# Values products of attention one half step later, beside the scores of a later unit

## The reference, cut to what matters

```python
# x: attention output, (2304 tokens, 512); batch 4, 8 heads, seq 576, head_dim 64
scores = scale * np.matmul(q, k.transpose(0, 1, 3, 2))
mask_local = (rel >= 0) & (rel < stride)                    # heads 0 to 3, stride 32
mask_strided = (rel >= 0) & (pos[None, :] % stride == pos[:, None] % stride)   # heads 4 to 7
scores = np.where(masks[None, :, :, :], scores, -1000000000.0)
attn = np.exp(scores - np.max(scores, axis=-1, keepdims=True))
attn = attn / (np.sum(attn, axis=-1, keepdims=True) + 1e-09)
x = np.matmul(attn, v)                                      # heads side by side
h = x @ w_in                                                # 512 to 2048
g = np.where(h >= 1, h, np.where(h <= -1, 0.0, (h + 1) ** 2 / 4.0))
y = g @ w_out                                               # 2048 to 512
out = y.copy()                                              # then, where y @ w_skip > 0:
e_idx = np.argmax(y @ w_gate, axis=1)                       # one of 8 experts
out += gate_w * (np.maximum(y @ w1[e_idx], 0.0) @ w2[e_idx])
```

## Time and profile before

| | |
|---|---|
| time, median of 3 runs (lowest to highest) | 545.35 us (545.23 to 545.76) |
| the profiled execution's own time | 546.15 us |
| its span | 541.5 us |
| mean granted TensorE clock | 0.973 of full speed |
| TensorE busy with matmuls | 520.1 us, 96% |
| VectorE, ScalarE, GpSimd busy | 250.2, 206.2, 211.6 us |
| chain that ended last, TensorE's share | 89% |

### The profile page before, as it was taken

One profiled execution on the slowest core, in us unless ns is written; L12 is line 12 of the kernel. 1 busy time (PEld: TensorE's weight loads), 2 busy tenths in 40 slices (PEclk: granted clock), 3 DMA queues, 4 the chain that ended last, 5 costly groups with the idle time before them and its releaser, 6 DMA issues.

```text
span 541.5 us, 9204 instructions
## 1 busy us (share of the span) xinstructions
PE 520.1 (96%) x3555; PEld 450.0 (83%) x3556; DVE 250.2 (46%) x585; ACT 206.2 (38%) x451; POOL 211.6 (39%) x242
## 2 busy tenths in 40 slices
PE   6889999999999999999999999999999999999993
PEld 3677888889998888888888888888899988898892
DVE  6956566533226435646535547452322573222221
ACT  4953655642322324443423443432332223322221
POOL 1656788762222324544533535552222333221220
PEclk9777999999999999999999999999999999999998
DMA  8991201003001104201210420000300081740003
GB/s 249 348 383 63 68 30 47 30 2 116 1 1 50 63 24 161 73 4 36 86 44 18 145 75 30 4 0 21 116 1 1 0 312 43 254 153 1 2 0 119
DMA packets 19298, 42.95 MB, mean 79 GB/s; under 512 B 2116, under 2 KB 3856, under 8 KB 19252
## 3 DMA queue, kind: packets, MB, share of 16 engines
q1 hardware_dynamic: 19124, 42.32, 22.9%
q0 software_dynamic: 128, 0.02, 0.0%
HBM read 33.01 MB, written 9.57 MB: 79 GB/s over the span
## 4 chain that ended last, share of the span: by engine, by line
PE 89%; DVE 6%; issue 1%; POOL 1%; DMA 1%; ACT 1%; SPq 0%; DVEq 0%; ACTq 0%; POOLq 0%
PE bank L957 37%; PE bank L973 34%; PE bank L832 4%; PE bank L796 4%; PE bank L813 3%; PE bank L850 2%; PE bank L842 1%; DVE row_sum L1116 1%; DVE bank L1099 1%; PE bank L986 1%; DVE row_max L1104 1%; PE bank L906 1%; DMA qk<-in_qk_dram 1%; PE bank L887 1%; DVE prob_first L1090 1%
## 5 line engine op out<-in xcount | busy, mean ns | idle before, releaser
L1685 POOL TENSOR_TENSOR g_lo<-act_f,g_hi 128x384 fp32r<-128x384 f32 x96 | 97.1, 1012 | 204.8 <-ACT g_hi L1571 204.4
L1562 ACT ACTIVATE act_f<-act_f,half_col 128x384 f32<-128x384 f32 x96 | 59.2, 617 | 209.3 <-DVE act_f L1314 209.1
L1314 DVE TENSOR_SCALAR act_f<-bank 128x384 f32<-128x384 f32 x96 | 53.3, 556 | 163.1 <-PE bank L957 160.9
L957 PE MATMUL bank<-x_hi,win_hi 128*128 128x384 f32 x384 | 91.7, 358 | 0.0
L1571 ACT CAST g_hi<-act_f 128x384 fp32r<-128x384 f32 x96 | 49.2, 512 | 94.6 <-DVE act_f L1317 94.2
L957 PE MATMUL bank<-x_hi,win_lo 128*128 128x384 f32 x384 | 85.1, 341 | 0.0
L973 PE MATMUL bank<-wout_hi,g_hi 128*128 128x512 f32 x282 | 84.9, 410 | 0.0
L957 PE MATMUL bank<-x_lo,win_hi 128*128 128x384 f32 x384 | 84.4, 339 | 0.0
L973 PE MATMUL bank<-wout_hi,g_lo 128*128 128x512 f32 x282 | 80.3, 393 | 0.0
L973 PE MATMUL bank<-wout_lo,g_hi 128*128 128x512 f32 x282 | 80.2, 393 | 0.0
L1317 DVE TENSOR_TENSOR act_f<-act_f,bank 128x384 f32<-128x384 f32 x96 | 52.3, 545 | 40.0 <-ACT act_f L1562 38.3
(11 more groups left out here) (131 smaller groups left out, 481.7 us busy)
## 6 DMA issues: line engine op xcount, KB each, us to landing
w_early<-in_w_dram SPq DMA_DIRECT2D x4, 2048.0 KB, 9.1
qk<-in_qk_dram SPq DMA_DIRECT2D x12, 592.0 KB, 4.0
out_dram<-y_rows SPq DMA_DIRECT2D x18, 256.0 KB, 2.6
y_dram<-y_rows SPq DMA_DIRECT2D x18, 256.0 KB, 2.8
win_raw<-in_w_in_dram SPq DMA_DIRECT2D x16, 256.0 KB, 9.7
wout_raw<-in_w_out_dram SPq DMA_DIRECT2D x16, 256.0 KB, 9.8
v<-in_v_dram SPq DMA_DIRECT2D x6, 384.0 KB
v<-in_v_dram SPq DMA_DIRECT2D x6, 288.0 KB
```

The lines of the kernel that those rows point to most:

```text
L957: mm = pe.matmul(h_ps[s % 2][:, 0:CH], w[:, f, P * k:P * (k + 1)], x[:, k, cols], start=(at == 0), stop=(at == len(order) - 1))
L1314: dve.tensor_scalar(tile, h_ps[s % 2][:, 0:CH], -1.0, 1.0, ALU.max, ALU.min).then_inc(clip_ready, 1)
L1562: act.activation(tile, tile, ACT.Square, bias=half_col[:, 0:1], scale=0.5).then_inc(square_ready, 1)
L1685: pool.tensor_tensor(g_lo[:, s % RING, :], act_f[:, s % 2, :], g_hi[:, s % RING, :].bitcast(F32), ALU.subtract).then_inc(g_lo_ready, 1)
```

## The change

In c = 2 and 3 the last argument of `unit_at`, the distance of a unit's V from its S in half steps, goes from 5 to 6. Everything else follows from the list: the half step in which all engines do their part of V, SyncE's load behind it, and the order in which banks are dealt out.

```diff
--- before.py
+++ after.py
@@ -132,7 +132,7 @@
             unit_at(N_PRO + REST + i, 18 + 4 * (i - EARLY), 5, 7)
     if c in (2, 3):
         for i in range(PER_BATCH):
-            unit_at(N_PRO + REST + PER_BATCH * (c - 1) + i, 1 + 3 * i, 4, 5)
+            unit_at(N_PRO + REST + PER_BATCH * (c - 1) + i, 1 + 3 * i, 4, 6)
     if c == EARLY_CHUNKS:
         for i in range(5):
             got[19 + i].append(("rank", i))
```

## The result

| | before | changed |
|---|---|---|
| median of 20 runs each (lowest to highest) | 545.01 us (543.65 to 546.23) | 546.97 us (544.36 to 548.77) |
| profiled execution, its span | 546.15 us, 541.5 us | 547.22 us, 542.9 us |

The ratio is 1.0031, with a 95% interval of 1.0017 to 1.0046: slower by 0.9 to 2.5 us. The predicted time was 546.2 us, 0.85 us above the median of 545.35 us that it started from.

The account below looks back on a forecast made before the run. TensorE's queue in its written order was taken to bound the kernel. Per chunk -1.1 - 0.36 + 1.9 = +0.44 us, twice +0.9, giving a median of 546.2 us, range 545.0 to 547.9.

Parts of the forecast that it names:

- the queue: TensorE's blocks in written order, chunks three and four: their length plus new waits, +0.44 us a chunk, +0.9 in all.
- Fewer block changes: TensorE, six units a chunk: V beside S pays one pair of 0.09 us instead of two, -1.1 us a chunk.
- the value in the middle: TensorE, V straight into S: the step costs 0.09 us, as leaving V does now, already contained in 0.65.
- rival D: TensorE, V into S: a dear step, 0.17 us more at eight places, +1.4 us, 547.6 in all; chance 0.16.
- x_lo off unit 7's path: VectorE, unit 7's row sums no longer stand behind V(6)'s x_lo; TensorE's wait goes, -0.36 us a chunk.
- The bank that comes free too late: Half steps 7 and 13: Y and Z wait for V's bank, 1.03 and 0.87 us, +1.9 a chunk.
- the restart: TensorE in half steps 7 and 13: the waiting block starts 0.14 us after V's bank is released.
- The allowance of up to 0.3 each for other engines: Half steps 7 and 13: ScalarE or VectorE still busy could lengthen each new wait by 0 to 0.3 us.
- A wait of this size doesn't cost the clock: TensorE, the new waits: the granted clock stays at 1.00, as beside a 1.51 us wait before 529.93; no cost.
- Rival B: Half steps 7 and 13: no new bank wait, only the gains, -2.9 us, so 542.4; chance 0.08.
- Rival C: VectorE: x_lo ahead of S's masking delays Y and Z in half steps 11 and 17, +1.4 us, 547.6; chance 0.16.
- The spare time: Half steps 11 and 17: 0.35 us of additional delay fits before masking queued behind x_lo holds up Y or Z.

Follow-up runs that it names:

- e1_after: The changed kernel run again, against the kernel before: 545.84 us, ratio 1.0012 (0.9994 to 1.0029).
- e7_four_units: Only V(1), V(3), V(4) and V(5) moved a half step later, against the kernel before: 543.94 us, ratio 0.9977.
- e6_unit6: Only V(6) moved, from half step 24 to 25, against the kernel before: 544.81 us, ratio 0.9992.
- e4_six_units: All V but V(0) and V(2) moved a half step later, against the kernel before: 542.34 us, ratio 0.9948.

## Why the prediction was right, and where not

The measured time, 546.97 us, lies in the range of 545.0 to 547.9, and slower was the likeliest outcome by the chances (0.48). In part that was luck: the queue, which was all that the sum held, gives +0.3 us, and what lifted the first comparison to about +2 us is a cost that the prediction had ruled out. The single forecast of +0.9 us was half of what came there and about what e1_after gave (+0.8). Step by step:

- **Fewer block changes, -1.1 us a chunk**: right. Four units gave 0.76 us (e7_four_units), 0.19 for each. V into S costs 0.65 in all, the value in the middle; rival D is out. The Trainium skill (TensorEngine Tiling (Array Packing), Key Properties) says that a change of tiling mode drains the engine, and gives no price; the 0.65 agrees with it, since this change costs as much as V to o did.
- **x_lo off unit 7's path, -0.36**: right, 0.37 (e6_unit6).
- **The bank that comes free too late, +1.9**: right in mechanism and place, 0.2 too large. The waits cost 0.91 and 0.76, where 1.03 and 0.87 stood. The term that was mis-sized is the restart: 0.14 us taken from a wait for GpSimd; after VectorE's x_lo it is 0.05, and x_lo took 0.66 and not the 0.70 below which it could hardly fall. The allowance of up to 0.3 each for other engines wasn't needed.
- The three make +0.2 us a chunk; chunk three measured +0.15. **The queue as a whole**: +0.3 us for both chunks instead of +0.9. Had nothing else happened, the kernel would have been unchanged within what can be measured.
- **"A wait of this size doesn't cost the clock"**: wrong. This is the step that failed. It rested on one wait of 1.51 us at the end of one trace and the 1.00 beside it. That stretch ends at 530, 0.07 us after the wait, and so can't show what follows it; the next one of the same trace does, and it was at 1.00 too:

```profile
530.00:535.00 5.00, 4.30 (x18) 3.20 (x18) 1.96 (x5) 1.17 (x2) 0.00 (x0) 1.00 0.20 76
```

So the observation holds, though not by the row given for it; what failed is the step from that wait to these. Waits of 0.83 and 0.69 us, a good 19 us apart, were followed by 3.4 us at half the clock in four of six passes of the kept traces, at 1.5 us each. Why it is always the wait of half step 13 and never that of 7, why in some passes only, and why the longer wait at the end is followed by none, the runs don't show. By the estimate from all executions the falls add 0.3 to 1.4 us to an average one of the changed kernel; with the queue's 0.3 that is 0.6 to 1.7 us.
- Rival B (no wait) is out by the rows of the waits. Rival C (scores behind x_lo on VectorE) is out by e7_four_units and e4_six_units: TensorE shows no wait ahead of L842 and L850 in half steps 11 and 17. The spare time was small but enough (3.99 - 3.60 = 0.39 us by the prediction's own figures, where it says 0.35).

## What to carry to other kernels

When a job moves in a schedule written out by hand, write down the order in which buffers are dealt out in the new half step, and look for a pair in it whose distance is a multiple of the ring: that pair waits for the whole way from full to free. On an engine that is never idle, price a new wait twice, once for its own length and once for the clock that may fall behind it, and leave out the moves that bring such a wait: here two of eight, which turned a change of +0.1 to +0.3% into one of -0.4 to -0.5%.

## What the runs showed of the hardware

A wait of TensorE under 1 us in a stretch that was busy otherwise can be followed by about 3.4 us at a granted clock of 0.50, though TensorE is fully busy again by then. The same waits filled with matmuls whose results nobody reads were not followed by that in any of four passes. A filled pass was 1.4 us shorter than one with a fall and 0.13 longer than one without. The times of the filled kernels show no gain beyond their noise. A wait of 1.5 us ahead of the last outputs, which eleven of the twelve kept traces have, was in none followed by a fall while the last outputs ran.

Sixteen matmuls more in TensorE's program took 2.3 us off the time without touching the chunks (542.54 to 540.26), all of it outside the profiled span (4.67 to 1.79 us; the span of that one execution was 2.4 us longer, 2.0 of it before its first `hidden` block, which is the variation of the beginning told above; the mean spans are 538.6 and 538.3). The cause is open.
